# The fullest expert goes first, and its first three tiles run while the last 256 rows are routed

## The reference

```
logits = y @ w_gate                      # 8 columns
e = argmax(logits); gate = softmax(logits)[e]
out[row] = gate * (relu(y[row] @ w1[e]) @ w2[e])     # w1: 512x1024, w2: 1024x512
```

## Time and profile before

| | us |
|---|---|
| median of 3 runs | 1280.41 (1278.49 to 1280.99) |
| the profiled execution | 1278.91 |
| its span, first to last instruction | 1277.2 |
| PE busy | 1213.2 (95%) |
| DVE busy | 745.3 (58%) |
| ACT busy | 632.8 (50%) |
| POOL busy | 522.3 (41%) |
| mean TensorE clock granted | 0.978 of full speed |

### The profile page before, as it was taken

The page is one execution under the profiler, slowest core; times in us unless marked ns, Lnnn a source line. Parts: engine busy times, 40 slices in busy tenths (PEclk is TensorE's granted clock), DMA queues, the critical chain, the costliest instruction groups (busy, mean ns, idle before and its releaser), DMA issues.

```text
span 1277.2 us, 20438 instructions
## 1 busy us (share of the span) xinstructions
PE 1213.2 (95%) x6740; PEld 961.1 (75%) x6741; DVE 745.3 (58%) x1018; ACT 632.8 (50%) x1088; POOL 522.3 (41%) x379
## 2 busy tenths in 40 slices
PE   6799999999999999999999965999999999999995
PEld 4577777877777777777778744888888888888884
DVE  4698788788887888878887765050500023282400
ACT  3556666666665666566654532333333333333332
POOL 3244234244243442434424232454544455555543
PEclk8899999999999999999999987999999999999998
DMA  8200301103003020020200206142411123353311
GB/s 261 67 20 1 67 3 47 23 1 67 3 9 61 1 67 3 1 67 1 77 24 4 96 18 222 42 133 82 141 66 41 41 89 123 113 168 102 104 35 37
DMA packets 74655, 80.71 MB, mean 63 GB/s; under 512 B 52063, under 2 KB 52063, under 8 KB 73570
## 3 DMA queue, kind: packets, MB, share of 16 engines
q1 hardware_dynamic: 55506, 59.80, 16.3%
q0 software_dynamic: 7568, 20.03, 4.7%
q10 hardware_dynamic: 11520, 0.09, 0.5%
HBM read 61.70 MB, written 19.49 MB: 64 GB/s over the span
## 4 chain that ended last, share of the span: by engine, by line
PE 80%; DVE 6%; POOL 5%; ACT 3%; DMA 3%; issue 2%; ACTq 0%; POOLq 0%; SPq 0%; DVEq 0%
PE ps L1002 72%; PE ps L1281 3%; POOL g_lo L480 2%; PE ps L1244 1%; DMA sread<-x_rows,take 1%; POOL xx L456 1%; POOL xx L451 1%; PE ps L1075 1%; PE ps L1019 1%; DVE u L904 1%; DVE u L897 1%; PE ps L1046 1%; ACT th L600 1%; DMA take<-expert_tokens 1%; DVE u L901 1%
## 5 line engine op out<-in xcount | busy, mean ns | idle before, releaser
L1002 PE MATMUL ps<-W,A 128*128 x1872 | 448.6, 395 | 2.8 <-ACT A L715 1.3
L1002 PEld LDWEIGHTS ps<-W,A 128*128 128x128 f32 x1872 | 347.4, 189 | 73.5 <-issue 3.8
L480 POOL TENSOR_TENSOR g_lo<-u,g_hi 128x512 fp32r<-128x512 f32 (+1 forms) x144 | 186.8, 1297 | 435.7 <-ACT g_hi L607 404.2
L1002 PE MATMUL ps<-wout,g_hi 128*128 128x512 f32 x1088 | 339.2, 393 | 0.4 <-POOL g_lo L480 0.4
L1002 PEld LDWEIGHTS ps<-wout,g_hi 128*128 128x128 f32 x1088 | 204.2, 188 | 43.8 <-POOL g_lo L480 1.1
L1002 PE MATMUL ps<-A,G 128*128 128x512 f32 x768 | 210.3, 409 | 4.4 <-issue 2.5
L1002 PE MATMUL ps<-wout,g_lo 128*128 128x512 f32 x544 | 212.4, 390 | 0.0
L889 DVE CAST W<-xn 128x1024 fp32r<-128x1024 f32 x28 | 21.5, 769 | 303.6 <-PE ps L1002 302.7
L904 DVE COPY_PREDICATED u<-big,th 128x512 f32<-128x512 uint8 (+1 forms) x144 | 179.7, 1248 | 23.4 <-DVE u L901 23.1
L1002 PEld LDWEIGHTS ps<-A,G 128*128 128x128 f32 x768 | 135.7, 189 | 67.9 <-issue 39.8
L599 ACT ACTIVATE u<-ps 128x512 f32<-128x512 f32 (+1 forms) x144 | 82.7, 574 | 118.1 <-PE ps L1002 97.9
(11 more groups left out here) (154 smaller groups left out, 1211.9 us busy)
## 6 DMA issues: line engine op xcount, KB each, us to landing
xn<-in_moe_w SPq DMA_DIRECT2D x32, 512.0 KB
xn<-in_x SPq DMA_DIRECT2D x32, 256.0 KB
x_rows<-xx SPq DMA_DIRECT2D x8, 1024.0 KB
spare<-in_moe_w SPq DMA_DIRECT2D x16, 512.0 KB
sp<-in_moe_w SPq DMA_DIRECT2D x16, 512.0 KB
win<-in_moe_w_in SPq DMA_DIRECT2D x4, 1024.0 KB, 11.2
Araw<-in_moe_w_out SPq DMA_DIRECT2D x6, 512.0 KB, 6.2
spare<-in_moe_w_out SPq DMA_DIRECT2D x2, 512.0 KB, 6.0
```

Source lines behind the costliest of these rows:

```text
L480: nc.gpsimd.tensor_tensor(g_lo[:, c % GR, 0:n], u[:, c % 2, 0:n], g_hi[:, c % GR, 0:n], ALU.subtract).then_inc(g_lo_made, 1)
L1002: return nc.tensor.matmul(o, l, r, start=start, stop=stop)
```

## The change

Before the last 256 rows are known, the kernel counts the rows of each expert in the first seven batches (3584 rows, so the fullest has at least 448, more than three tiles), takes the fullest and lets it change places with expert 0. The order of the experts is then `order`, and the expert at position 0 has three tiles that are settled whatever the last rows bring. Everything that went by expert number (slots, tiles, loads) goes by position; DRAM addresses go by `order`.

- **DVE** (`choose_order`): 17 operations, each waiting for the one before, in batch 7 after chunk 10, then `order_ready`. In the table of tiles, five operations more to exchange two counts and one more on the starts. Chunks 4 to 7 of the first expert are split right after the last dense chunk, ahead of the routing of batch 8.
- **PE**: one product for the early counts in batch 7, chunk 9; a wait for the order in batch 8, chunk 4; the turn of tile 0's rows in batch 8, chunk 13, into bank P0. The results of batch 8 go to two other banks. After the dense part, gemm1 of tiles 0 and 1 and gemm2 of tile 0 stand between the steps of the routing; `tables_ready` is awaited after them.
- **ACT**: loads numbers and gates of tile 0 in batch 8, chunk 2, and the numbers of tile 1 at chunk 12, and makes `xe` of tile 0 at chunk 14. All four remaining high parts of the first expert come before the copies of the last rows. The wait for `table_written` stands before the load of tile 3.
- **POOL**: gathers tile 0 in batch 8, chunk 10. After the dense part: `xe_lo(0)`, gather 1, `xe_lo(1)`, gather 2, `he_lo(0)`, and only then `enter(8)` and the wait for the stores.
- **SP**: writes zeros to the eight places of state rows in DRAM, after `load_x(1)`; loads the first expert's chunks after `order_ready`, at an address read from `order_i`.
- `xg` lies in `Araw[:, 3072:3584]` instead of the `sread` buffer, and `passed` and `skipped` in `xx`.

```
@@ pool, in the loop over chunks
+                if t == B and f == 10:
+                    pool.wait_ge(h_done, FC * B)
+                    pool.wait_ge(zero_row_stored, 16 * (1 + B))
+                    pool.wait_ge(x2_stored, 16 * B)
+                    gather(0)
...
-            enter(B, range(SR // P))
...
-            pool.wait_ge(x2_stored, 16 * (B + B))
-            pool.wait_ge(zero_row_stored, 16)
-            gather(0)
             xe_lo_of(0)
             regather(1)
             xe_lo_of(1)
             regather(2)
             he_lo_of(0)
+            enter(B, range(SR // P))
+            pool.wait_ge(x2_stored, 16 * (B + B))
@@ act, in the loop over chunks and after it
+                if t == B:
+                    if f == 2:
+                        act.wait_ge(order_ready, 1)
+                        act.wait_ge(table_written, 16 * (1 + C * EARLY))
+                        load_take(0, first=True, starts=early_start)
+                        load_put(0, first=True, starts=early_start)
...
+                    if f == 12:
+                        load_take(1, starts=early_start)
+                    if f == 14:
+                        xe_copies(0, first=True)
             g_hi_of(FC * (B + 1) - 1, SR)
-            expert0_hi(range(ECH, ECH + 2))
+            expert0_hi(range(ECH, ECHUNKS))
             y_copies(B, SR // P)
             act.wait_ge(x2_turned, C * B + 1)
...
+            logits_copy(B, LT_last)
             relu(0)
             xe_copies(1)
-            load_take(2)
+            load_take(2, starts=early_start)
+            gate_exp(B, SR // P)
             he_copies(0, first=True)
             relu(1)
             xe_copies(2)
+            act.wait_ge(starts_ready, 1)
+            act.wait_ge(table_written, 16 * (1 + NT))
             load_take(3)
@@ dve
+            def choose_order():
+                mx, fe = first_e[:, 0:1], first_e[:, 1:2]
+                rows = P0[:, 0:E]
+                dve.wait_ge(early_counts_done, 1)
+                link(nc.vector.tensor_reduce(mx, rows, AX.X, ALU.max))
+                link(nc.vector.tensor_tensor(pick[:], rows, mx.to_broadcast([P, E]), ALU.is_equal))
...
+                nc.vector.tensor_copy(early_start[:], early_f[:]).then_inc(order_ready, 1)
...
+                if t == EARLY and f == 10:
+                    choose_order()
...
+            for i in range(ECH, ECHUNKS):
+                split_chunk(0, 0, i, hi_by_act=True)
             dve.wait_ge(x2_turned, NT)
@@ pe
+                if t == EARLY and f == 9:
+                    pe.wait_ge(onehot_made, EARLY)
+                    mm(P0[:, 0:E], ones[:], seen[:, C, :], True, True).then_inc(early_counts_done, 1)
+                if t == B and f == 4:
+                    pe.wait_ge(order_ready, 1)
+                if t == B and f == 13:
+                    turn_rows(0, P0)
...
             pe.sem_inc(he_done, 1)
             pe.sem_inc(tile_done, 1)
+            gemm1_hi(0, 0, (0, 1))
+            pe.wait_ge(xe_raw_made, 1)
+            pe.wait_ge(ranks_read, B)
+            for i in range(SR // P):
+                pe.wait_ge(y_copied, C * B + i + 1)
+                for k in range(K):
+                    last = nc.tensor.transpose(ps[:, 6 + i, P * k:P * (k + 1)], x2[:, i, P * k:P * (k + 1)], ident[:])
+                last.then_inc(x2_turned, 1)
+            gemm1_hi(0, 0, (2, 3))
+            pe.wait_ge(x2T_copied, C * B + 1)
+            pe.wait_ge(x2T_last_copied, 1)
+            for k in range(K):
+                last = mm(P0[NS * k:NS * (k + 1), 0:SR], wg[:, k, :], x2T[:, 2:4, k, :], True, True)
+            last.then_inc(logits_done, 1)
+            gemm1_lo(0, 0)
+            turn_logits(B, LT_last, SR // P)
+            turn_rows(1, PXT)
+            turn_h(0)
+            gemm1_hi(1, 0, (0, 1))
+            pe.wait_ge(logits_made, B + 1)
+            ranks(B, SR // P)
+            mm(P0[:, 0:E], ones[:], seen[:, C, :], True, True).then_inc(counts_done, 1)
+            gemm1_hi(1, 0, (2, 3))
+            gemm1_lo(1, 0)
+            turn_rows(2, PXT)
+            gemm2(0, 0)
+            turn_h(1)
+            pe.wait_ge(tables_ready, 1)
@@ sp
+            for b in range(B):
+                sp.dma_start(x2_dram[b * T + S:(b + 1) * T, :], LT_buf[0:NS, :]).then_inc(zero_row_stored, 16)
...
             sp.wait_ge(stage_done, STAGES * B)
             wait_split(sp, 5)
+            sp.wait_ge(order_ready, 1)
+            e = expert_at(0)
             for i in range(RING):
-                sp.dma_start(raw_as(i, raw[i]), expert_chunk(0, i)).then_inc(raw_loaded[i], 16)
+                sp.dma_start(raw_as(i, raw[i]), expert_chunk_at(e, i)).then_inc(raw_loaded[i], 16)
             store_x2(B - 1)
```

More of the change, by code:

```diff
@@ L633, in expert0_hi, with xe_copies, relu, he_copies @@
                     nc.scalar.copy(slot_hi(0, i), raw[i % RING]).then_inc(e0_hi_made, 1)
+            def xe_copies(j, first=False):
+                bank = P0 if first else PXT
+                act.wait_ge(xe_turned, j + 1)
+                if not first:
+                    act.wait_ge(xe_lo_made, j)
+                nc.scalar.copy(xe_hi.rearrange("p k s -> p (k s)"), bank).then_inc(xe_hi_made, 1)
+                nc.scalar.copy(xe_raw, bank).then_inc(xe_raw_made, 1)
+            def relu(j):
+                act.wait_ge(he_done, j + 2)
+                nc.scalar.activation(h_rows.rearrange("p (b n) -> p b n", b=2), PHE, ACT.Relu).then_inc(relu_done, 1)
+            def he_copies(j, first=False):
+                act.wait_ge(he_turned, j + 1)
+                if not first:
+                    act.wait_ge(he_lo_made, j)
+                nc.scalar.copy(he_hi, PHT).then_inc(he_hi_made, 1)
+                nc.scalar.copy(h_raw.rearrange("p (k s) -> p k s", k=KE), PHT).then_inc(he_raw_made, 1)
+            def y_scale(j, first=False):
+                act.wait_ge(tile_done, j + 2)
+                act.wait_ge(put_loaded, 16 * (j + 1))
+                nc.scalar.activation(y_rows, PYE, ACT.Copy, scale=put[:, 1:2].bitcast(F32)).then_inc(y_scaled, 1)
+            def table_rows(j, starts):
+                r = act.value_load(starts[0:1, ds(j, 1)], min_val=0, max_val=TABLE - P)
+                return table[ds(r, P), :]
+            def load_take(j, first=False, starts=tile_start):
+                if not first:
+                    act.wait_ge(gathered, 16 * j)
+                act.dma_start(take[:], table_rows(j, starts)).then_inc(take_loaded, 16)
+            def load_put(j, first=False, starts=tile_start):
+                if not first:
+                    act.wait_ge(scattered, 16 * j)
+                act.dma_start(put[:], table_rows(j, starts)).then_inc(put_loaded, 16)
             for st in range(4):
@@ L718, in y_scale @@
-            def y_scale(j, first=False):
-                act.wait_ge(tile_done, j + 2)
-                act.wait_ge(put_loaded, 16 * (j + 1))
-                nc.scalar.activation(y_rows, PYE, ACT.Copy, scale=put[:, 1:2].bitcast(F32)).then_inc(y_scaled, 1)
-            def table_rows(j):
-                r = act.value_load(tile_start[0:1, ds(j, 1)], min_val=0, max_val=TABLE - P)
-                return table[ds(r, P), :]
-            def load_take(j, first=False):
-                if not first:
-                    act.wait_ge(gathered, 16 * j)
-                act.dma_start(take[:], table_rows(j)).then_inc(take_loaded, 16)
@@ L733, in load_put @@
[L733 to L746 removed]
+            nc.scalar.copy(x2T[:, 2, :, :], P0.rearrange("p (k s) -> p k s", k=K)).then_inc(x2T_copied, 1)
@@ L1264, in gemm1 @@
                 last.then_inc(he_done, 1)
+            def gemm1(j, e):
+                gemm1_hi(j, e, range(K))
+                gemm1_lo(j, e)
             def gemm2(j, e):
```

225 lines of the change are left out of this document (109 added, 116 removed).

## The result

The changed kernel takes **1265.27 us** (median of four runs, 1263.37 to 1265.85) against 1280.12 for the kernel before beside it (1278.49 to 1280.99): a ratio of 0.9883 [0.9866, 0.99], 14.85 us less. The profiled execution took 1263.37.

What follows compares the result with a forecast made beforehand. PE bounds the kernel, with some 30 us of waits and half clock before the loop. 26.2 us earlier less a 2.5 stall is 23.7, taken as 23.4: span 1253.8, median 1257.0, range 1251 to 1265.

Steps and rivals of the forecast that it cites:

- Their numbers are asked for at 764.2, there 1.7 to 3.9 us later: After the dense part: load of tile 2's row numbers, with its gather then beginning at 766.3 to 768.1.
- granted clock 1.00 from 751 to 790: Sign expected in the profile after: PE keeps its full clock from the dense part's end into the expert loop.
- What bounds the kernel, and where the gain lies: PE bounds; between dense part and loop lie 47.2 us, some 30 of them waits and half clock, all that can be won.
- the passage: First matmul of gemm1(0) to gemm1 of tile 3; forecast there: gemm2(0) 26.2 us earlier, less a 2.5 us stall.
- 0.63 us a tile: Rival "slower", 3%: gathered rows in A's space cost each of 37 loop tiles; this cost decides, 0.8 would give 1287.
- ends 3.5 us late: Dense part, batches 7 and 8 together: its end moves 3.5 us later, to 754.7.
- 1.2 to 4.5: Batch 7: range of the cost, 3.0 us, of the early counts on PE and of choosing the order on DVE.
- Batch 8 "0.5": Batch 8: early loads, gather and turn of tile 0 together cost 0.5 us, up to 2.
- gemm2(0) at 772.2: After the dense part: gemm2 of tile 0 starts at 772.2 against 798.39, 26.2 us earlier.
- A new stall of 2.5 us, 0 to 4: PE waits for tile 3's rows, needed at 784.0, because the last rows' entries stand on POOL behind he_lo(0).
- numbers 780, its gather begins 781: Tile 3: entries written 776, numbers at 780, gather from 781 beside four weight chunks, landing 785 to 788.
- the waits come back: Rival, 22%: both late gathers slow, dense part loses 4.5, clock lost before gemm2(0), 2.7 us more; about 1265.

Runs made afterwards that it cites:

- the choice in batch 8: Changed kernel, but early counts taken at chunk 0 and the order chosen at chunk 1 of batch 8, not in batch 7: 1262.27 us, ratio 0.986.
- the early ask: Changed kernel, but ACT asks for tile 2's numbers ahead of tile 0's relu and the copies of tile 1's rows: 1253.91 us, ratio 0.9797.
- the entries first: Changed kernel, but POOL scatters the last rows' entries right after tile 2's gather, ahead of he_lo of tile 0: 1261.94 us, ratio 0.9855.
- holding the clock: Changed kernel plus spare PE transposes, 24 ahead of tile 2's rows and 40 ahead of tile 3's: 1265.39 us, ratio 0.9882.
- the two that hold the weights back in halves: Changed kernel, tile 2's numbers asked earlier, entries before he_lo(0), second expert's weights held until tile 3's, then tile 4's rows: 1258.78 us; with order chosen in batch 8, 1255.80.
- the one that holds them back whole: Changed kernel, but SP issues all eight of the second expert's weight chunks only after tile 3's rows have landed: 1258.83 us, ratio 0.984.

## Why the prediction was right and wrong

**The step that failed.** "Their numbers are asked for at 764.2, there 1.7 to 3.9 us later": the 1 KB load was priced without the 2 MB of weights issued just ahead of it, and it took 5.6 us. At tile 3 the same term, 1 us in the working, took 4.65. With it fell "granted clock 1.00 from 751 to 790". The edit that moves only the first of these requests takes away both waits, both falls of the clock and 11.4 us.

**What bounds the kernel, and where the gain lies: right.** 18.2 us came out of the passage; nothing came from anywhere else. The loop's tile is 12.25 of 12.25 us as before (12.29 in the trace of the same kernel run again), far from the 0.63 us a tile at which the move of the gathered rows into A's space would have decided, and no wait for rows stands at chunk 13 of batch 8.

**The dense part "ends 3.5 us late": 3.9** (batch 7 had "1.2 to 4.5"; its terms add to 1.7 + 3 = 4.7). Made as foreseen: the wait for the counts (1.17), two for DVE's g (0.91, 1.19), one operation held by POOL. The experiment with the choice in batch 8 gives 3.0 us back in the median, 3.6 in the trace. Batch 8 "0.5": 0.3.

**gemm2(0) at 772.2: 772.16, right for two wrong reasons.** The numbers took 5.6 us, from an ask at 761.74. I had written of the 2 MB of weights that they lie beside the *rows*; they lay ahead of the *numbers*, whose price I took from rows with less in flight (in the row of 3.95 us the third chunk was issued at 767.49, after the ask at 766.13). It cost a wait of 3.00 us where the working has 0.7. That the date still held is luck: it is due to the dense part's end at 752.7 instead of 754.7, in a trace whose start was 2.4 us quick. From gemm1(0) to gemm2(0) it is 19.4 us against 17.5 predicted; with the early ask 17.0 (756.45 to 773.46).

**"A new stall of 2.5 us, 0 to 4": 4.67**, outside its bounds. The place, and that the entries stand on POOL behind he_lo(0), were right. They go out at 771.92 and 773.25, 6.2 us after DVE has the places (765.7) and still ahead of the working's 776, and the numbers are asked for at 779.36, on its date. What failed comes behind that: the numbers take 4.65 us where the working has 1 ("numbers 780, its gather begins 781"), so the gather starts at 784.82, and the rows take 5.63 more.

**"Granted clock 1.00 from 751 to 790": failed, and it is the largest single term in the trace.** The granted clock fell to its lower level, 1.2 GHz, twice. gemm2(0) and gemm2(1) took 7.31 and 7.91 instead of 5.71, 1.6 and 2.2 us; with the slower turn before the second, over 4 us. My reason against it was a wait of 1.9 us that left the clock at 1.00, this row of the kernel before:

```profile
789.72 0.66 PE L1244 MATMUL ps<-ident,sread 128*128 128x128 f32 x4 [1.90 <-DMA sread<-x_rows,take]
```

It said nothing of waits of 3 and 4.7 us, and the sum I made contained one of 2.5. The rival "the waits come back" (22%) had a loss of clock with its price, and its 1265 is what was measured, but partly by luck: it has both gathers land as slowly as the one of 6.54 us, while tile 2's took 3.5 and was late because of its numbers, and it counts one fall of the clock (2.7) where two came (1.6 and 2.2). The Trainium skill (TensorE: Matmul & The Clock Gate, HAM oscillation) states that a pause for DMA can put the clock back to half each time it recurs; this trace agrees, with two waits and two falls. In the kernel with the entries first, the wait of 3.51 us was not followed by a fall.

**The miss, added up.** The passage was to shrink by 27.2 (gemm2(0) 29.7 earlier, counted from the end of the dense part, less 2.5) and shrank by 18.2: 9.0 missing, of which 1.9 by tile 2's rows, 2.2 by tile 3's, 4.3 by the clock (1.6, 2.2 and 0.45 in the turn), and 0.6 not accounted for. With 0.4 in the dense part, 1.1 late in the loop, and 2.4 the other way by the start, that is 8.1 against the 7.8 by which the trace's span missed its 1253.8; the 0.3 between them is the prediction's own rounding, 23.7 taken as 23.4. The experiment that asks earlier has a passage of 36.21: 29.6 shorter than before, more than the forecast, with one wait of 0.60 us for rows and none at tile 3. **So what the change does was right, the price of one small load was not, and the forecast lay between two versions that differ by one line's place.**

**Still open.** In the changed kernel's trace a wait of 0.60 us for the weights and a few tenths beside it appear late in the loop, at 1138.12. The trace of the same kernel run again does not have them, and yet its stretch behind the passage is as long (461.32 against 461.34 us): its tiles take 12.29 us instead of 12.25 from the start of the loop on. What sets these 0.04 us a tile no run shows. And holding the clock by itself changed nothing in the median.

## What to carry to other kernels

When a change lets work start earlier, list the small requests on which the next step hangs, and look what bulk transfer each queue issues in the 2 us ahead of them: a 1 KB load is priced by what is in flight, 1.7 us or 5.6 to 6.9 here, and the first late one goes on through every in-order queue behind it. Ask for the small thing first; holding the bulk back only moved the collision here. And price a new wait of some 3 us on TensorE as the wait and, in a second sum, half-clock work behind it: here 7.7 us of waits and 4.3 of clock.

## What the hardware showed that was not expected

- A load of 1 KB took 1.7 us with nothing beside it or with its bulk load still to come, and 5.6 to 6.9 us when another engine had begun to issue 2 MB 1.2 to 2.3 us ahead of it (5.6 and 6.0 in the two traces of the changed kernel, 6.9 in that with the clock held). In the changed kernel the chain shows 4 us of it as "issue", which names no cause.
- The length of a wait does not alone decide over the clock: at the passage it fell behind 3.00, 3.12 and 3.48 us, stayed up behind 3.51, and fell behind 1.43 in that same trace; it fell behind 1.67 and 2.05 in the two that hold the weights back in halves, and stayed up behind 2.04 in the one that holds them back whole. What tells these apart the runs do not show.
- The start is worth up to some 5 us from run to run with no change in it: up to the mark in batch 6 the traces read between 626.28 and 631.83. In a wait of batch 0 the clock fell in ten traces (3.30 to 3.37 us; 16 matmuls behind it take 1.96 us) and stayed up in three (2.98 to 3.27; 1.09). The first attention product, too, starts at 14.23 us in the changed kernel's trace and at 17.16 in that with the entries first. A single trace can therefore be compared only from a mark inside it.
